# A decay-attention, expert and SoLU kernel on one core: w loaded first from two queues, paddings cleared by VectorE, the first diagonal put by two engines, state updates ahead of the scores

## What is computed

```python
# attention with decay, per batch and head; w and u have one value per head and channel
for t in range(S):
    cur = outer(u * k[t], v[t])
    y[t] = r[t] @ (state + cur)
    state = w[:, None] * state + outer(k[t], v[t])
x = y as rows of 384 (8 heads x 48), 1536 tokens
# experts: each token goes to the expert with the largest logit (8 experts, 384 slots each)
e = argmax(x @ w_gate);  x = gate_w * (relu(x @ w1[e]) @ w2[e])
# SoLU layer
h = x @ w_in;  s = h * softmax(h);  out = (layernorm(s) * g_ln) @ w_out
```

## Time and profile before

| | us |
|---|---|
| median of 3 runs | 333.94 |
| lowest and highest | 333.18, 336.49 |
| the profiled execution | 335.37 |
| its span | 333.3 |
| TensorE busy in it | 314.3 (94%) |
| VectorE, ScalarE, GpSimd busy | 207.4, 197.0, 189.2 |

### The profile page before, as it was taken

How to read it: one execution, slowest core, us unless ns; L and a number is a source line. 1 busy time by engine, 2 the same in 40 slices (tenths; PEclk the granted TensorE clock), 3 DMA queues, 4 the chain that set the end, 5 groups by cost and what they waited for, 6 DMA issues and landing times.

```text
span 333.3 us, 6568 instructions
## 1 busy us (share of the span) xinstructions
PE 314.3 (94%) x2382; PEld 282.1 (85%) x2382; DVE 207.4 (62%) x475; ACT 197.0 (59%) x377; POOL 189.2 (57%) x172
## 2 busy tenths in 40 slices
PE   6799998988799999999999999899999999999991
PEld 2688887866699999999999999788999999999991
DVE  4657758796835555464646464889897666656610
ACT  2578786774565858576766676466556445533520
POOL 6976689871675989888797969700031111111131
PEclk9999999999989999999999999999999999999998
DMA  8999999992594949393938486000000000000010
GB/s 129 161 284 262 242 244 255 269 387 83 160 388 145 317 122 346 108 347 120 318 138 286 172 242 250 5 0 3 1 26 24 24 26 24 24 26 25 26 41 30
DMA packets 62898, 50.65 MB, mean 152 GB/s; under 512 B 42512, under 2 KB 58256, under 8 KB 62864
## 3 DMA queue, kind: packets, MB, share of 16 engines
q1 hardware_dynamic: 58896, 45.25, 47.3%
q0 software_dynamic: 1920, 4.73, 3.9%
q10 hardware_dynamic: 2048, 0.22, 0.7%
HBM read 38.37 MB, written 11.82 MB: 151 GB/s over the span
## 4 chain that ended last, share of the span: by engine, by line
PE 75%; POOL 6%; issue 5%; DVE 5%; ACT 3%; DMA 3%; POOLq 0%; DVEq 0%; ACTq 0%; SPq 0%
PE ps L1302 23%; PE ps L1596 15%; PE ps L1579 15%; PE ps L1303 11%; PE ps L1605 3%; ACT scores L749 2%; POOL own_place L551 2%; POOL own_place L555 2%; PE ps L1460 1%; PE ps L1438 1%; PE ps L1296 1%; DMA x_slots<-w_raw,slot 1%; DMA wsq<-in_w_dram 1%; PE ps L1375 1%; PE ps L1406 1%
## 5 line engine op out<-in xcount | busy, mean ns | idle before, releaser
L494 POOL TENSOR_TENSOR w_lo<-w_raw,w_hi 128x768 fp32r<-128x768 f32 x33 | 60.4, 1856 | 15.0 <-DVE w_lo L500 14.9
L1302 PE MATMUL ps<-xe,w_hi 128*128 128x448 f32 x192 | 63.3, 384 | 2.4 <-DVE h L942 2.1
L1302 PE MATMUL ps<-h,w_hi 128*128 128x448 f32 x192 | 61.6, 377 | 0.0
L1596 PE MATMUL ps<-w_hi,h 128*128 128x384 f32 x192 | 51.5, 340 | 0.0
L1303 PE MATMUL ps<-xe,w_lo 128*128 128x224 f32 x192 | 51.4, 268 | 0.0
L1303 PE MATMUL ps<-h,w_lo 128*128 128x224 f32 x192 | 50.8, 264 | 0.0
L648 POOL TENSOR_TENSOR rstd<-var_b,minus_half 128x1 f32<-128x1 f32 x12 | 6.8, 565 | 72.5 <-DVE var_b L1248 72.5
L1579 PE MATMUL ps<-w_hi,xe 128*128 128x512 f32 x144 | 46.4, 392 | 0.9 <-ACT xe L862 0.9
L935 DVE TENSOR_TENSOR ps<-ps,rk_in 128x448 f32<-128x448 f32 x32 | 20.2, 633 | 37.6 <-ACT rk_in L704 37.6
L1302 PEld LDWEIGHTS ps<-xe,w_hi 128*128 128x128 f32 x192 | 36.7, 191 | 7.6 <-issue 4.8
L500 POOL TENSOR_TENSOR w_lo<-w_raw,w_hi 128x1024 fp32r<-128x1024 f32 x16 | 38.1, 2402 | 2.9 <-DVE w_lo L500 2.9
(11 more groups left out here) (162 smaller groups left out, 615.1 us busy)
## 6 DMA issues: line engine op xcount, KB each, us to landing
w_raw<-in_moe_w_dram SPq DMA_DIRECT2D x15, 1536.0 KB, 7.7
x_slots<-zeros SPq DMA_DIRECT2D x6, 768.0 KB, 5.7
rk_in<-in_r_dram SPq DMA_DIRECT2D x12, 192.0 KB, 5.3
rk_in<-in_k_dram SPq DMA_DIRECT2D x12, 192.0 KB, 5.9
v_in<-in_v_dram SPq DMA_DIRECT2D x12, 192.0 KB, 5.9
out_dram<-zeros SPq DMA_DIRECT2D x1, 2304.0 KB, 8.1
w_raw<-in_moe_w_dram SPq DMA_DIRECT2D x3, 512.0 KB, 5.4
rows_in<-x_slots SPq DMA_DIRECT2D x8, 192.0 KB, 7.8
```

What stands on the lines that cost most here:

```text
L494: eng.tensor_tensor(w1_lo[:, :, cols], w1_raw[:, i, :, cols], w1_hi[:, :, cols].bitcast(F32), ALU.subtract).then_inc(g.w1_lo, 1)
L1302: pe.matmul(ps[:, bank, 0:2 * n], w_hi, x[:, c, 0:2 * n], start=first, stop=False, skip_group_check=True)
L1596: last = pe.matmul(ps[:, OB + i, 0:DM], ht[:, f, i * P:(i + 1) * P], wt[:, f, :], start=(f == 0 and z == 0), stop=(f == KF - 1 and z == 2))
```

## The change

Five edits. (1) The two halves of w go out from two queues, the odd heads by SyncE ahead of all its tiles and behind `wcol_ready`, the even heads by ScalarE. (2) The paddings of `rk_in` and `v_in` are cleared by VectorE behind `pick_pair`, no longer by GpSimd; k_last's stays. (3) The first diagonal's odd half is put by VectorE, with four tensor_scalar products right behind own(0), and has a semaphore of its own; ScalarE puts the even half only. (4) The counts in the waits on `diag_ready` follow from that (`diagonals(t)`). (5) From tile 1 on `state_update(t)` stands ahead of `key_query(t)`.

```diff
@@ sync
+            sp.wait_ge(wcol_ready, 1)
+            load_w(sp, 1)
             for t in range(NB):
                 load_tile(t)
@@ helpers
+        def diagonals(t):
+            return max(2 * t - 1, 0)
+        def load_w(eng, g):
+            eng.dma_start(wsq[DP * g:DP * g + D, 0, :, 0], w.rearrange("(p g) d -> g d p", g=2)[g],
+                          allow_slow_non_contiguous=True).then_inc(w_dma, 16)
@@ gpsimd
-            pool.memset(rk_in[:].rearrange("p a b h d -> p (a b h) d")[:, :, D:DP], 0.0).then_inc(pads_ready, 1)
-            pool.memset(v_in[:].rearrange("p a h d -> p (a h) d")[:, :, D:DP], 0.0).then_inc(pads_ready, 1)
@@ scalar
-            w_pairs = w.rearrange("(p g) d -> g d p", g=2)
-            for g in range(2):
-                act.dma_start(wsq[DP * g:DP * g + D, 0, :, 0], w_pairs[g],
-                              allow_slow_non_contiguous=True).then_inc(w_dma, 16)
+            load_w(act, 0)
...
                 if t > 0:
                     take_y(t - 1)
-                put_diagonal(t, 1)
+                    put_diagonal(t, 1)
@@ vector
             dve.memset(pick_pair[:], 0.0).then_inc(pick_step, 1)
+            dve.memset(rk_in[:].rearrange("p a b h d -> p (a b h) d")[:, :, D:DP], 0.0).then_inc(pads_ready, 1)
+            dve.memset(v_in[:].rearrange("p a h d -> p (a h) d")[:, :, D:DP], 0.0).then_inc(pads_ready, 1)
...
                 if t > 0:
-                    dve.wait_ge(diag_ready, 2 * t)
+                    dve.wait_ge(diag_ready, diagonals(t))
                 dve.tensor_reduce(own[:], ruk[:], AX_X, ALU.add).then_inc(own_ready, 1)
+            def put_first_diagonal():
+                dve.wait_ge(own_ready, 1)
+                for p in range(HP):
+                    last = dve.tensor_scalar(scores[:, 0, 1, p, :], ident[:], own[:, 2 * p + 1:2 * p + 2], None, ALU.mult)
+                last.then_inc(first_odd_ready, 1)
...
-                    dve.wait_ge(diag_ready, 2 * t + a + 1)
+                    if t == 0 and a == 1:
+                        dve.wait_ge(first_odd_ready, 1)
+                    else:
+                        dve.wait_ge(diag_ready, diagonals(t) + a + 1)
...
             add_own(0)
+            put_first_diagonal()
@@ tensor
             for t in range(NT):
                 b, c = divmod(t, NC)
+                if t > 0 and c < NC - 1:
+                    state_update(t, (NC - 1) * b + c)
                 key_query(t)
-                if c < NC - 1:
-                    state_update(t, (NC - 1) * b + c)
+                if t == 0:
+                    state_update(0, 0)
```

More of the change, by code:

```diff
@@ L300, in decay_attention_moe_solu @@
         scattered = sem("scattered")
+        first_odd_ready = sem("first_odd_ready")
         key_ready = sem("key_ready")
```

## The result

The changed kernel took 337.01 us at the median of 20 runs (334.38 to 338.82). The kernel before, on the same chip, took 333.8 us over 20 runs (331.8 to 336.49). The ratio is 1.0087, 95% interval 1.0066 to 1.0109: the change makes the kernel 0.9% slower. A second set of 12 runs, beside 35 of before, gave 336.0 us against 334.09 us, ratio 1.0053 [1.0020, 1.0086]. The two intervals overlap between 1.0066 and 1.0086, so I count 2 to 3 us of loss. The forecast was 335.7 us, in 332.4 to 338.6.

A forecast was written before the change was run, and what follows sets the result against it. The prediction took TensorE, fully busy in middle attention tiles, and SyncE's stream of tile loads, binding at tile 6, as the bounds. Start 0, stream +0.4 and tile 8 +1.4 on 333.94 gave 335.7 us, range 332.4 to 338.6.

The forecast's parts named there:

- The start.: Start of the kernel: w lands at 4.2, 1.0 us before 5.22; the gain ends at k(1) and k(6), counted 0.
- the smaller reading in the prediction: Start: two queues save only w's second issue, some 0.45 us, since all DMAs share the same 16 engines; sum unchanged.
- The stream, +0.4: SyncE's tile loads start later behind w, so k(6) and own(6) come late: +0.4 us, range -0.1 to +0.7.
- rival 1: Start: VectorE's four products each wait for a GpSimd product, masks at 16.2, +1.6 us, total 336.9; chance 0.12.
- Paddings.: Start: VectorE takes over the memsets of 1024 and 512 columns, ready near 4.0; cost 0, with 0.2 us cover.
- The reorder outside tile 8, costed at 0: Attention tiles: scores come 0.61 us later behind the update, absorbed by VectorE's slack; cost 0, up to 0.2.
- Tile 8, +1.4: Tile 8: update waits for the slots with scores queued behind, delaying tile 9's first diagonal: +1.4 us, bounds +0.5 to +1.87.
- The sum.: Whole kernel: start 0, stream +0.4, tile 8 +1.4, together +1.8 us, giving 335.7 us on the median of 333.94.
- Rival 2: SyncE's tile stream starts only once w has landed, making k(6) 2.6 us late, total 337.9; chance 0.10.
- Rival 3: The stream does not bind, so the start's gain at own(1), up to 1.0 us, survives, total 334.3; chance 0.12.
- Rival 4: Tile 8: slots no longer meet GpSimd's products, so the cost there is +0.5 us, total 334.8; chance 0.12.

The follow-up runs named there:

- profiles of the table: One profiled execution each of the kernel before, the changed kernel and their variants, some profiled twice; ratios to before 1.0004 to 1.0087.
- the first profile: Profiled execution of the unchanged changed kernel from its first set of runs: 336.41 us, span 334.7; that set's median 337.01 us, ratio 1.0087.
- not at tile 8: Changed kernel with the scores ahead of the state update at tile 8 alone, the update first at later and earlier tiles from 1 on: 335.38 us, ratio 1.0035.
- the first warmed profile: Changed kernel with eight warming matmuls on zeros ahead of tile 8's state update, first of two measurements: 337.02 us, ratio 1.0064.
- the tiles-first versions: SyncE's tile loads ahead of the x_slots zeroing, in the kernel before (338.15 us, ratio 1.0108) and in the change less the reorder (339.16 us, 1.0138).
- the last version above: Changed kernel with both halves of w issued by ScalarE and the scores first at tile 8 alone: 335.51 us, ratio 1.0046.
- the second profile of after: Changed kernel, unchanged, profiled again in the second set of runs: 336.0 us, ratio 1.0053, span 333.7.

## Why the prediction was right, and where its reasons were not

**The start.** The loads of w landed for GpSimd at 3.30; I had taken 4.2. The second issue alone, the smaller reading in the prediction, would have given 0.45 us; it was 1.92, with each half landing after 1.8 to 2.2 us instead of 2.6 to 3.7. Whether this is the second queue or w's place ahead of the tiles is not separated. VectorE was the later one, at its memsets until 3.4 (its first product with w began at 3.64). The step overlooked k(0). In all seven profiles of the table with half of w on SyncE, TensorE's first transposes begin at 7.58 to 7.83, each time behind a wait for that load; in the five others at 5.64 to 6.58. SyncE issued k(0) at 1.98 instead of 1.30, and in the first profile it landed at least 1.4 us later (7.72 for 6.28). So of the 1.92 us only 0.78 reached own(0). What was left ended at k(1), as I had reasoned: k(1) held GpSimd until 12.02, I had put it at 11.2 to 11.9, and own(1) moved by 0.02 in this execution.

**The stream, +0.4.** The size came out (own(6) 41.51, between 41.0 and 41.8), and the step was still incomplete. Own(6) varies from execution to execution when w goes by SyncE: 41.33 to 42.35 in six profiles with all of edit 1 to 3, against 41.04 and 41.09 in before. Own(8), which I had not followed, is 0.7 to 1.7 us late in five of them and 2.9 in the sixth. But it is 0.68 late with the reorder alone too, where w goes as before. In the two latest (not at tile 8, and the first warmed profile) GpSimd's first scatter waited 1.52 and 1.20 us for the zeroing of `x_slots`, which stands in the same queue of SyncE: the place where the tiles-first versions lost. The change less the reorder costs 0.33% [0.08, 0.59], some 1.1 us, so the term was nearer to +1 than to +0.4. That w's place on SyncE makes k(0) late is shown by the twelve profiles; that it is the cause of the 1.1 us was not separated: w by two queues alone gave 1.0016, the other two edits 1.0004, and neither differs from 1 for certain.

**VectorE's four products, rival 1.** The step said that GpSimd would leave VectorE a gap if it had to wait for k(1), and that without the gap the products would be blocked. Both are shown: 0.91 us with the gap, 2.49 to 2.85 without (2.49 in the last version above). The price was put too high. The products were to end at 14.69 and the masks at 16.2, 1.6 late; in the second profile of after they ended at 14.22 and 15.47, and own(1) was 0.86 behind the 15.10 of before.

**Paddings.** No cost found, as forecast.

**The reorder outside tile 8, costed at 0.** Wrong at tile 1. With the reorder alone own(2) follows own(1) by 5.20 us, without the reorder by 5.21, and with both the reorder and the odd diagonal on VectorE by 5.61 to 5.63, in all six such profiles. The update of tile 1 waits for the state that VectorE copies behind own(1), so the scores stand behind it; that is so with the reorder alone too, and there it costs nothing. The difference is that the masks start 1.69 us after the scores' first matmul, where 1.26 is usual (16.76 to 18.45 above, 56.32 to 57.58 in the second profile, and 16.88 to 18.14 with the reorder alone). Why these 0.43 us are there I don't know; it stays open. A late start of the same kind stands at tile 9 of the reorder alone (scores at 62.63, masks at 64.87), so it isn't bound to tile 1. The delay is carried to tile 5, and tile 6 takes a part of it back in some executions (4.98 us instead of 5.20).

**Tile 8, +1.4.** The mechanism is shown: TensorE's idle time of 1.76 to 2.32 us (I had said 1.8), the scores queued behind it, the masks late, and a loss of 1.31 to 1.33 us from own(8) to own(9) where the clock stayed. That is my +1.4. What my sum lacked was the clock, which it put at nothing. It fell behind this very gap in two of three executions and then added 1.34 us. I had spoken of such a stretch as part of what I don't see, and had not tied it to the gap that I was creating. A wait that is new on TensorE can have this second term.

**The sum.** I said +1.8; measured is +3.2 in the first set of runs and +1.9 in the second. The terms as the runs show them are about +1.1 for the first three edits, 1.3 at tile 8, and up to 1.3 for the clock in part of the executions. So the range held by its margin: the two missing sizes, some 0.7 for the first three edits and up to 1.3 for the clock, lie inside it. That 337.01 is close to the 336.9 of rival 1 is a coincidence, as its condition did not hold in the first profile and its price was not paid in the second. Rival 2, the queue held by w's packets, is false in its size: k(6) came 0.25 to 1.27 late in the six profiles, not 2.6. Rival 3, the surviving start, is false: own(1) is at 14.96 at the earliest in all profiles. Rival 4 is false: slots and GpSimd's product met in all twelve profiles of the table, where the first operation on the slots took 1.14 to 1.32 us.

## What to carry to other kernels

Before an instruction is moved up in an engine's queue, look up every semaphore that it waits for in every turn of the loop: here one turn of nine had one wait more, and it held all that stood behind it. Price such a gap on TensorE twice, once as the wait, and once as the lower clock that may follow. And a start that is won is worth only what the next transfer in line lets through; find the first load behind it that someone waits for, here k(0) and then k(1), and see whether the edit itself makes it later, before counting the gain.

## What was not expected of the hardware

The clock after a gap of about 2 us came out both ways. Gaps of 2.27 and 2.32 us were followed by about 3 us at 0.5 to 0.6, one of 1.76 by none; and a gap of 2.11 us by a low stretch in one execution and by full speed in another of the same kernel. The cost where it came was 1.34 us at tile 8, and the two spans of before differ by 1.9, of which 0.3 lies ahead of the gap. The mean of several profiles, or the medians, is needed to price it; one profile told half of the story.

Four VectorE products of 128 columns took 0.91 us while GpSimd stood idle for most of it, and 2.49 to 2.85 beside GpSimd's two-input products, so 1.6 to 1.9 us longer. The Trainium skill, SBUF — State Buffer, section Who interferes with whom, says that tensor_scalar can enter a mode on two ports, in which it and a GpSimd instruction block each other for a whole instruction. The durations here agree with that; which mode ran, the traces don't show.
